# A three-stage kernel on one core: the MLP takes its tokens in a new order, and its first block is fetched beside the last expert chunk

## The reference

```python
# experts: N, D, E, F = 1536, 512, 8, 1024
do_compute = x @ w_skip > 0
out = x.copy()
xc = x[do_compute]
logits = xc @ w_gate
e_idx = np.argmax(logits, axis=1)
gate_w = softmax(logits)[range(len(xc)), e_idx]
for e in range(E):
    mask = e_idx == e
    h = np.maximum(xc[mask] @ w1[e], 0.0)
    y[mask] = gate_w[mask, None] * (h @ w2[e])
out[do_compute] = xc + y
# MLP: w_in 512 x 2048, w_out 2048 x 512
h = x @ w_in
g = np.where(h > 0.0, h, np.exp(np.minimum(h, 0.0)) - 1.0)
return g @ w_out
```

## Time and profile before

| | us |
|---|---|
| median of 3 runs | 572.92 |
| lowest, highest | 572.15, 574.18 |
| the profiled execution | 573.41 |
| its span | 571.4 |
| mean granted clock of PE in it | 0.97 |

### The profile page before, as it was taken

How to read it: one execution, slowest core, us unless ns; L and a number is a source line. 1 busy time by engine, 2 the same in 40 slices (tenths; PEclk the granted TensorE clock), 3 DMA queues, 4 the chain that set the end, 5 groups by cost and what they waited for, 6 DMA issues and landing times.

```text
span 571.4 us, 8866 instructions
## 1 busy us (share of the span) xinstructions
PE 536.6 (94%) x3211; PEld 466.4 (82%) x3212; DVE 273.4 (48%) x706; ACT 211.5 (37%) x419; POOL 43.5 (8%) x98
## 2 busy tenths in 40 slices
PE   5999999998599999999479999999999999999997
PEld 3777777777399999999368999898998989989985
DVE  7565655553744144458436663433443344433332
ACT  3575655553033133346224532422233222332222
POOL 6000000000110000100320000110002000000000
PEclk9999999999589999999859999999999999999999
DMA  9188797323029659999471000110003000010001
GB/s 217 65 293 289 259 310 266 122 90 112 20 74 348 247 178 351 371 359 339 159 238 75 2 0 1 58 54 1 0 1 93 17 1 0 0 56 0 1 0 56
DMA packets 47943, 73.21 MB, mean 128 GB/s; under 512 B 16484, under 2 KB 16740, under 8 KB 47908
## 3 DMA queue, kind: packets, MB, share of 16 engines
q1 hardware_dynamic: 43570, 64.23, 32.8%
q0 software_dynamic: 1840, 6.03, 3.4%
q10 hardware_dynamic: 2498, 2.51, 1.3%
HBM read 58.08 MB, written 14.68 MB: 127 GB/s over the span
## 4 chain that ended last, share of the span: by engine, by line
PE 91%; DVE 4%; issue 2%; DMA 2%; ACT 1%; POOL 0%; POOLq 0%; DVEq 0%; ACTq 0%
PE ps_g L1257 24%; PE ps_out L1257 23%; PE ps_h L1468 12%; PE ps_y L1257 9%; PE ps_pv L1348 7%; PE ps_qk L1278 5%; PE ps_turn L1304 4%; PE ps_turn L1330 2%; PE ps_pv L1360 1%; DVE prob L972 1%; PE ps_x L1487 1%; PE ps_x L1437 1%; PE ps_turn L1312 1%; DMA row_sb<-slots,slot_i 1%; DMA xg<-tokens,source_i 1%
## 5 line engine op out<-in xcount | busy, mean ns | idle before, releaser
L1257 PE MATMUL ps_g<-x_hi,w_hi 128*128 128x384 f32 x256 | 87.6, 342 | 1.5 <-DVE x_lo L1219 1.5
L1257 PE MATMUL ps_g<-x_lo,w_hi 128*128 128x384 f32 x256 | 87.2, 341 | 0.0
L1257 PE MATMUL ps_g<-x_hi,w_lo 128*128 128x384 f32 x256 | 87.1, 340 | 0.0
L885 ACT ACTIVATE g_raw<-ps_g 128x384 f32<-128x384 f32 x64 | 31.5, 492 | 129.8 <-PE ps_g L1257 129.6
L1227 DVE TENSOR_SCALAR g_raw<-g_raw 128x384 f32<-128x384 f32 x64 | 23.1, 361 | 116.3 <-ACT g_raw L885 114.3
L1257 PE MATMUL ps_out<-w_hi,g_hi 128*128 128x512 f32 x192 | 75.5, 393 | 0.6 <-DVE g_lo L1235 0.6
L1257 PE MATMUL ps_out<-w_lo,g_hi 128*128 128x512 f32 x192 | 75.9, 395 | 0.0
L1257 PE MATMUL ps_out<-w_hi,g_lo 128*128 128x512 f32 x192 | 75.6, 394 | 0.0
L1468 PEld LDWEIGHTS ps_h<-xg_t,up_w 128*128 128x128 f32 x576 | 67.7, 197 | 2.0 <-issue 1.3
L1468 PE MATMUL ps_h<-xg_t,up_w 128*128 128x128 f32 x576 | 68.0, 280 | 0.9 <-ACT xg_t L835 0.9
L889 ACT ACTIVATE g_hi<-g_raw 128x384 fp32r<-128x384 f32 x64 | 33.7, 526 | 62.3 <-DVE g_raw L1230 62.3
(11 more groups left out here) (144 smaller groups left out, 688.5 us busy)
## 6 DMA issues: line engine op xcount, KB each, us to landing
raw<-in_moe_w SPq DMA_DIRECT2D x16, 1024.0 KB, 7.2
up_w<-in_moe_w SPq DMA_DIRECT2D x16, 1024.0 KB
raw<-in_moe_w_in SPq DMA_DIRECT2D x4, 1024.0 KB, 6.8
raw<-in_moe_w_out SPq DMA_DIRECT2D x4, 1024.0 KB, 6.5
slots<-zeros SPq DMA_DIRECT2D x2, 1792.0 KB, 9.5
v_pad<-in_v SPq DMA_DIRECT2D x16, 192.0 KB, 5.0
tokens<-x_tok SPq DMA_DIRECT2D x6, 512.0 KB, 4.5
out_tokens<-row_sb SPq DMA_DIRECT2D x12, 256.0 KB, 2.1
```

The source lines that it names most:

```text
L885: act.activation(g_raw[f % GB][:], ps_g[f % 2][:, 0:TW], ACT.Exp).then_inc(g_exp_done, 1)
L1257: last = pe.matmul(to, w, x, start=start and m == 0, stop=stop and m == 2)
```

## The change

The order in which the MLP takes the tokens, and where x and the gate are added, are new.

- There is one table in DRAM, `rows_dram`: first the slots, then the tokens, then zeros. The row of a token with an expert is its slot, that of a token without one is its own x. So `inactive` is now the row of the token's x instead of a number beyond the slots.
- The experts write finished rows: `y_sb` becomes gate x `ps_y` + x in one DVE operation. The gates of a chunk's slots are picked by 12 bf16 matmuls into `ps_gates` after the first transposes (`gates_as`, three bf16 parts of each gate). The x of the chunk is kept by a new ACT copy, `x_keep<-xg`, at the head of each chunk. `xg` may be overwritten only after it (`xg_kept`), so POOL gathers one chunk ahead instead of two. The store of chunk g moves from the end of ACT's chunk g to the head of chunk g+1.
- The first 9 tiles of tokens (`ET`) are put into a new order by class: no expert first, then expert 0, 1, and so on. DVE finds the classes in four steps after `sources` column 0; PE sums places in 18 matmuls (`ps_place`, then `ps_list` in 18 more after expert 0); DVE's `place_tokens` runs before its chunk 0. The result `lists` holds for each tile the rows to gather and the tokens to which the output goes. The last three tiles keep the order of the tokens (`late_rows`).
- The first tile of that order is gathered in the place of one more chunk (`sources` column `end`), and transposed by the last chunk's `turn`. Tiles 1 and 2 are gathered after it, without a wait for the stores. In the first `up` of the first block the eight matmuls that need only `x_hi` come first.
- Output of the nine tiles goes by POOL's indirect scatter; only the last block is stored by SP. `combine` is gone.
- The loop over pairs of experts on PE has its first pair written out.

```diff
-    slots_dram = nc.dram_tensor("slots", [SLOTS + 2 * P, D], F32, kind="Internal").ap()
-    tokens_dram = nc.dram_tensor("tokens", [N + P, D], F32, kind="Internal").ap()
-    token_tiles = tokens_dram.rearrange("(t p) d -> p t d", p=P)
-    slot_chunks = slots_dram.rearrange("(c p) d -> c p d", p=P)
+    rows_dram = nc.dram_tensor("rows", [SLOTS + N + P, D], F32, kind="Internal").ap()
+    token_tiles = rows_dram[SLOTS:SLOTS + N].rearrange("(t p) d -> p t d", p=P)
+    slot_chunks = rows_dram[0:SLOTS].rearrange("(c p) d -> c p d", p=P)
...
+        ps_x2 = [psum(f"ps_x2{i}", [P, DC, P]) for i in range(TB)]
+        ps_x = ps_x2[0]
+        ps_list = ps_x2[1][:].rearrange("p c k -> p (c k)")[:, 0:2 * ET]
+        ps_place = ps_x2[2][:].rearrange("p c k -> p (c k)")[:, 0:ET * E1].rearrange("p (t e) -> p t e", e=E1)
...
-            with sp.Fori(0, NB) as tb:
-                for i in range(TB):
-                    sp.wait_ge(out_copied, tb * TB + i + 1)
-                    sp.dma_start(out_tiles[bass.ds(tb * TB + i, 1)].rearrange("o p d -> (o p) d"),
-                                 row_sb[i][:]).then_inc(out_stored[i], 16)
             for i in range(TB):
-                sp.wait_ge(out_stored[i], 16 * NB)
+                sp.wait_ge(out_copied, ET + i + 1)
+                sp.dma_start(out_tiles[ET + i], row_sb[i][:]).then_inc(last_stored, 16)
+            sp.wait_ge(last_stored, 16 * TB)
+            for i in range(TB):
+                sp.wait_ge(out_stored[i], 16 * (NB - 1))
...
                 if not (isinstance(k, int) and k == 0):
                     pool.wait_ge(xg_turned, k)
+                    pool.wait_ge(xg_kept, k)
+                    pool.wait_ge(y_stored, (k + FREE - TB * 2) * 16)
...
             pool.wait_ge(all_named, 1)
-            gather_chunk(1)
             for e in range(E):
                 first, hi = bases
-                gather_chunk(first + 2)
+                if e == 2:
+                    pool.wait_ge(lists_ready, 1)
+                gather_chunk(first + 1)
                 with pool.If(first + 1 < hi):
                     with pool.Fori(first + 1, hi) as g:
-                        gather_chunk(g + 2)
+                        gather_chunk(g + 1)
                 if e + 2 < E1:
                     bases = [hi, base_of(pool, e + 2)]
             end = bases[1]
-            pool.wait_ge(y_stored, end * 16 + 16)
-            pool.wait_ge(xg_loaded, end * 16 + 32)
-            pool.wait_ge(xg_copied, end + 1)
-            pool.wait_ge(idle_done, end + 2)
+            def gather_tile(t):
+                index = lists[:, t:t + 1] if t < ET else late_rows[:, t - ET:t - ET + 1]
+                pool.indirect_dma_start(
+                    out=row_sb[t % TB][:], out_offset=None, in_=rows_dram[:, :],
+                    in_offset=bass.IndirectOffsetOnAxis(ap=index, axis=0),
+                    bounds_check=SLOTS + N, oob_is_err=False,
+                ).then_inc(gathered[t % TB], 16)
+            def scatter_tile(t):
+                pool.wait_ge(out_copied, t + 1)
+                pool.indirect_dma_start(
+                    out=out[0:ET * P, :], out_offset=bass.IndirectOffsetOnAxis(ap=lists[:, ET + t:ET + t + 1], axis=0),
+                    in_=row_sb[t % TB][:], in_offset=None, bounds_check=ET * P - 1, oob_is_err=False,
+                ).then_inc(out_stored[t % TB], 16)
+            for t in range(1, TB):
+                gather_tile(t)
+            pool.wait_ge(y_stored, (end + FREE) * 16)
+            pool.wait_ge(idle_done, end + 1)
             pool.tensor_tensor(idle[:], idle[:], idle[:], ALU.subtract).then_inc(idle_done, 1)
...
+            for i in range(TB):
+                if i:
+                    pool.wait_ge(x2_turned, i)
+                gather_tile(TB + i)
+            for tb in range(NB - 1):
+                for i in range(TB):
+                    scatter_tile(tb * TB + i)
+                if tb + 2 < NB:
+                    for i in range(TB):
+                        pool.wait_ge(out_stored[i], 16 * (tb + 1))
+                        gather_tile((tb + 2) * TB + i)
...
+            def store_rows(g):
+                act.dma_start(slot_chunks[bass.ds(g, 1)].rearrange("o p d -> (o p) d"),
+                              y_sb[:]).then_inc(y_stored, 16)
+            def chunk(g, hook, first=False):
+                act.wait_ge(y_copied, g + 1)
+                if not first:
+                    store_rows(g - 1)
+                act.activation(x_keep[:], xg[:], ACT.Copy).then_inc(xg_kept, 1)
                 for i in range(2):
                     act.wait_ge(up_done, g * 2 + i + 1)
                     act.wait_ge(down_done, g + 1)
                     hook(i)
                 turn_in(g + 1)
...
                 hook(2)
-                act.wait_ge(y_copied, g + 2)
-                act.dma_start(slot_chunks[bass.ds(g, 1)].rearrange("o p d -> (o p) d"),
-                              y_sb[:]).then_inc(y_stored, 16)
                 hook(3)
...
                 for i in range(TB):
-                    act.wait_ge(x2_turned, tb * TB + i + 1)
+                    if not (isinstance(tb, int) and tb == 0 and i == 0):
+                        act.wait_ge(x2_turned, tb * TB + i)
                     act.activation(x_hi[:, :, i * P:(i + 1) * P], ps_x2[i][:], ACT.Copy).then_inc(x2_hi_done, 1)
...
             high_rows(0)
+            act.wait_ge(y_copied, end + 1)
+            store_rows(end - 1)
...
-            dve.tensor_scalar(inactive[:], skip, 0.0, float(SLOTS), ALU.is_le, ALU.mult)
+            dve.scalar_tensor_tensor(out=inactive[:], in0=skip, scalar=0.0, in1=token_row[:],
+                                     op0=ALU.is_le, op1=ALU.mult)
...
+            ordered = chain(order_step)
+            of_class = [P, ET, E1]
+            ordered(dve.tensor_tensor(in_class[:], hot_b[:, 0:ET, :], class_e[:].broadcast_to([P, ET, E]), ALU.mult))
+            ordered(dve.tensor_reduce(class_of[:].rearrange("p t o -> p (t o)"), in_class[:], AX_X, ALU.add))
+            ordered(dve.tensor_tensor(member[:], class_no[:].broadcast_to(of_class), class_of[:].broadcast_to(of_class),
+                                      ALU.is_equal))
+            ordered(dve.tensor_tensor(lower[:], class_no[:].broadcast_to(of_class), class_of[:].broadcast_to(of_class),
+                                      ALU.is_gt))
+            assert CLASSED == 4
...
+            dve.wait_ge(list_step, 9)
+            gate = gates[:].rearrange("p (t o) -> p t o", o=1)
+            ordered(dve.tensor_copy(gate_parts[:, 0], gate))
+            ordered(dve.tensor_tensor(gate_rest[:], gate, gate_parts[:, 0], ALU.subtract))
+            ordered(dve.tensor_copy(gate_parts[:, 1], gate_rest[:]))
+            ordered(dve.tensor_tensor(gate_parts[:, 2], gate_rest[:], gate_parts[:, 1], ALU.subtract))
+            dve.tensor_tensor(gates_as[:], in_chunk[:].broadcast_to([P, 3, NT, CHUNKS]),
+                              gate_parts[:].broadcast_to([P, 3, NT, CHUNKS]), ALU.mult).then_inc(gates_named, 1)
...
+            def place_tokens():
+                dve.wait_ge(places_ranked, 1)
+                ordered(dve.tensor_tensor(placed[:], ps_place, member[:], ALU.mult))
+                ordered(dve.tensor_reduce(at_place[:].rearrange("p t o -> p (t o)"), placed[:], AX_X, ALU.add))
...
+                for m in range(2):
+                    ordered(dve.tensor_tensor(listed_as[:, m], in_tile[:].broadcast_to([P, ET, 2, ET]),
+                                              parts[:, m].broadcast_to([P, ET, 2, ET]), ALU.mult))
+                for t in range(ET):
+                    dve.tensor_scalar(there[:, t, :], lane[:, 0, :], lane_in[:, t, :], None,
+                                      ALU.is_equal).then_inc(there_ready, 1)
+                dve.tensor_copy(late_rows[:], slot[:, ET:, :].rearrange("p t o -> p (t o)"))
...
+            def keep_gates():
+                dve.wait_ge(gates_summed, 1)
+                dve.tensor_reduce(gate_slot[:], ps_gates[:, 0:3 * CHUNKS].rearrange("p (m c) -> p c m", m=3), AX_X,
+                                  ALU.add).then_inc(gates_kept, 1)
+                dve.wait_ge(gates_kept, 1)
+            def keep_lists(end):
+                dve.wait_ge(lists_summed, 1)
+                dve.tensor_copy(lists[:], ps_list).then_inc(lists_copied, 1)
+                dve.wait_ge(lists_copied, 1)
+                dve.tensor_copy(sources[:, bass.ds(end, 1)], lists[:, 0:1]).then_inc(lists_ready, 1)
...
-                dve.wait_ge(y_stored, g * 16 + 16)
-                dve.tensor_copy(y_sb[:], ps_y[:]).then_inc(y_copied, 1)
+                dve.wait_ge(y_stored, (g + FREE) * 16)
+                dve.wait_ge(xg_kept, g + 1)
+                dve.scalar_tensor_tensor(out=y_sb[:], in0=ps_y[:], scalar=gate_slot[:, bass.ds(g, 1)], in1=x_keep[:],
+                                         op0=ALU.mult, op1=ALU.add).then_inc(y_copied, 1)
...
+            place_tokens()
+            keep_gates()
...
```

(47 more changed lines are left out.)

169 lines of the change are left out of this document (105 added, 64 removed).

## The result

The changed kernel is slower, by 1.0%: 579.29 us median of 4 runs (577.5 to 581.43) against 572.59 for the kernel before, run beside it, a ratio of 1.0104 (95% interval 1.0086 to 1.0122). The forecast was 571.4, its range ended at 578.0. The profiled execution took 581.43 us, its span is 579.6 against 571.4: 8.2 us to account for, of which about 2 are above the median of the runs.

The account below looks back on a forecast made before the run. The matmul engine, busy 94% of the span, was taken as the bound, so only its waits or lower clock could be won. Terms -12.4 - 2.2 + 1.8 + 0.9 + 7.7 + 2.7 = -1.5 gave 571.4 us, range 563.5 to 578.

Parts of the forecast that it names:

- Handover and start of the MLP: Last `ps_y` to `ps_g`: 14.23 us becomes 1.85 (-12.4); the first two `up` groups: 7.08 becomes 4.83 (-2.2).
- The wait of `ps_out` for the low half: MLP's first block: one warm group of 2.09 us covers the 2.68 us from exp to `ps_out` short by 0.65.
- Routing: Before chunk 0: added DVE steps and gate work start `ps_h` at 159.35 instead of 157.55, +1.8 us (1.2 to 2.8).
- List matmuls: After expert 0: eighteen list matmuls stand in PE's path, +0.9 us (0.5 to 1.2).
- Waits for the rows: Chunks: PE's transposes wait for later-issued row gathers, +7.7 us (0 to 12); with the last chunk +10.4.
- Last chunk: ACT splits a weight piece before the store and copy, so the gather lands late: +2.7 us (0.8 to 4).
- rival (c): Clock falls in the chunks' waits, five `ps_h` take 9.53 us instead of 7.14, costing 12 us: 583 us; chance 0.05.
- Rival (b): Gathers beside weight loads take 6.2 us or more, PE waits in five chunks: 576.6 us; chance 0.30.

Follow-up runs that it names:

- e3: Changed kernel with `up_w` loads for experts 2 to 7 cut to one of 128 partitions: 568.51 us, ratio 0.9929.
- e4: Changed kernel with ten overwritten identity matmuls ahead of the transposes in every chunk, keeping PE busy where it waited: 581.7 us (one run).
- e1: Changed kernel with the transposes of the next chunk's rows moved between the two halves of `ps_y`: 564.63 us, ratio 0.9852.
- e5: Kernel before plus only the copy to `x_keep` and its release, gathering one chunk ahead instead of two: 596.17 us, ratio 1.0403.
- e7: Changed kernel with the transposes behind three quarters of `ps_y` and POOL's constants in the old order: 563.19 us, ratio 0.983.
- e8: As e7, with class steps after the gates, places and `place_tokens` after expert 0, list matmuls after expert 1: 563.37 us, ratio 0.9843.

## Why the prediction was wrong

- **Handover and start of the MLP: right.** 1.70 us against 1.85, 5.14 against 4.83. The wait of `ps_out` for the low half that I named is there.
- **Routing: right**, +2.1 for +1.8, `ps_h` at 160.27 for 159.35. Beside it, and unforeseen, stand 0.6 us by which attention ends later and the 0.7 of chunk 0's longer `ps_h`. I had let POOL's new constants cost nothing, because they end long before POOL's first copy; what they delay is a DVE operation of the attention (below).
- **List matmuls: half.** The matmuls take 0.61 us, less than forecast. But 1.01 us of issue follow before the next `ps_h`, which takes 7.38 instead of 7.14. In it PE's sequencer loads the next expert's chunk bounds. I had priced the matmuls by their busy time, and not what a break in the loop does to PE's queue.
- **Waits for the rows: right in total (11.3 for 10.4), wrong in form.** I assumed one landing of 5.45 us in five chunks. The rows show 6.0 to 6.7 in one and 3.4 to 4.0 in the next, so four waits of 1.6 to 3.2 us and three of 0.4. The sum of the waits hardly minds; the clock does.
- **Last chunk: right size, wrong reason.** I took the split's place, T+1.45, from the earlier trace rows; after, its piece had landed earlier and it ran from T-0.99 to T+1.02, ahead of the copy. The wait of 3.21 us there came from the ordinary relay, a landing of 6.1 and 0.63 us in POOL's index copy, and e3 repeats it. No run shows the forecast mechanism.
- **The clock in the waits: the step that failed.** I gave rival (c) 0.05 since in the gap of the earlier trace rows the clock had held for some 3 us of idleness, and took this as a licence for waits below 3 us. That row tells when the fall is seen, not what is enough to cause it. After, the fall comes 3.7, 3.2 and 2.3 us after PE stopped, with PE working again in two of the three: a wait of 2.46 us has already earned it. Rival (c) had a wrong price too, five chunks of `ps_h` at the lower level, 12 us. I had read the 9.53 us of the earlier trace rows as a `ps_h` at that level, while the granted clock there was 0.50 for the first 4.5 us alone. What is hit is the `ps_y` behind the wait, 1.4 to 2.2 us each, and two groups of transposes: 5.7 us for which the sum had nothing. e4 gets them back.
- **The transposes behind a wait.** 0.66 us for 0.44, 1.6 us in all, had no term either. It was not the clock that made them longer.
- **Sum.** The clock (5.7), these transposes (1.6) and the small terms at the start and in the lists (2.4) carry the time beyond the range; the waits alone do not. That the total of the waits came out near the forecast is in part luck, as it is made of other waits than I summed. Rival (b) at 576.6 had five waits near 2.3 us, closest to what the slow gathers did, and left the clock out as well.
- **Not explained:** the MLP is 1.2 us shorter (four blocks, 67.9 us each instead of 68.2). In the chain after a number of `ps_out` groups read 2.04 us where before has 2.09. No experiment was made on it.

## What to carry to other kernels

A wait of PE costs more than its length once it is long enough for the clock to fall, and a row of idle time doesn't show that part: look at the granted clock of the stretch behind the wait and at the duration of the same matmuls in other chunks. When a buffer's release moves from one engine's step to the end of a relay, the remedy is often not a faster relay but where the consumer stands: here four transposes, moved behind work that was there anyway, turned +1.0% into -1.5% (e1). Price a landing by the DMA share at its own place, and do not average over places where the share differs.

## What the runs showed of the hardware

**The clock can fall after the wait is over.** Waits of PE and what followed: 0.57, 1.56 and 1.65 us left it at 1.00; those of 2.46 us and more (2.46, 2.84 and 3.21 in the changed kernel, 2.98 in e3, 2.52, 2.63, 3.34 and 4.34 in e5) came with a stretch at 0.50. No run has a wait between 1.65 and 2.46 us in its chunks. In the changed kernel it began 3.7, 3.2 and 2.3 us after PE had stopped, and lasted 3.4, 3.4 and 6.8 us.

**DVE and POOL stop each other, in both directions.** At the start the changed kernel makes four more constants on POOL, so the long iota starts at 7.62 us instead of 7.24. Timelines of the kernel before, then of the changed one, then of e7:

```profile
7.24 0.78 POOL L643 IOTA rel<- 128x768 f32 x1
7.75 0.41 DVE L950 TENSOR_SCALAR bias<-far,limits 128x256 f32<-128x256 f32 x1 [0.62 <-issue]
```

```profile
7.62 0.80 POOL L685 IOTA rel<- 128x768 f32 x1
7.74 0.82 DVE L1023 TENSOR_SCALAR bias<-far,limits 128x256 f32<-128x256 f32 x1 [0.62 <-issue]
```

```profile
7.22 0.78 POOL L685 IOTA rel<- 128x768 f32 x1
7.73 0.41 DVE L1023 TENSOR_SCALAR bias<-far,limits 128x256 f32<-128x256 f32 x1 [0.62 <-issue]
```

The DVE operation starts at the same time in all three and ends 0.14 to 0.16 us after POOL's iota does: 8.16 behind 8.02, 8.56 behind 8.42, 8.14 behind 8.00. So 0.4 of the 0.6 us by which the experts start late are most likely four small constants on POOL: the reduction into `top` that opens the routing starts at 144.6 to 145.3 us in the five other runs with the new order and at 143.8 and 144.3 in e8 and e7 with the old one (144.78 in the changed kernel, 144.18 before), and that start moves by some 0.6 us among runs that have the same attention. The other direction is in the last chunk after, POOL's index copy beside DVE's split:

```profile
285.65 0.81 POOL L748 COPY source_i<-sources 128x1 int32 x1 [11.80 <-ACT x_keep L910]
```

```profile
285.19 1.22 DVE L530 TENSOR_TENSOR w_lo<-raw,w_hi 128x1024 fp32r<-128x1024 f32 x1
```

The copy takes 0.81 us instead of its usual 0.18 and ends at 286.46, behind DVE's 286.41. The Trainium skill (SBUF — State Buffer, "Who interferes with whom") says that the two share one pair of ports as an exclusive lock, for those instructions that use it: a DVE operation in a mode with two ports, or one with two inputs in SBUF against a POOL instruction that reads SBUF. Whoever issues first then blocks the other. The trace agrees both times, with 0.41 and 0.63 us; that the first DVE operation runs in such a mode is not shown by it. With the constants back in the old order, e7 has the first one's 0.41 us again; for the second no run took the split away, but e3's last chunk has the same 0.81 us beside the same split.
